# An attention and two-layer kernel: transposed tails moved behind the scores, reciprocal broadcasts re-ordered, a rounding moved from ScalarE to GpSimd, copies put ahead of exponentials

## What is computed

```python
# attention: 4 batches x 8 heads, 576 positions, head size 64
scores = q @ k.T / sqrt(64)
scores = where(scores >= max(scores) - tau, scores, -1e9)
attn = exp(scores - max(scores)); attn = attn / (sum(attn) + 1e-9)
x = attn @ v                      # heads side by side: 2304 tokens x 512
# two layers, each 512 -> 2048 -> 512
h = x @ w_in;  g = h * tanh(softplus(h));      x = g @ w_out
h = x @ w_in2; g = h * clip(h + 3, 0, 6) / 6;  out = g @ w_out2
```

## Time and profile before

| | |
|---|---|
| median of 3 runs | 1034.86 us (1034.7 to 1036.05) |
| the profiled execution, its own device time | 1034.37 us |
| its span, first to last instruction | 1032.6 us |
| PE busy | 1007.6 us, 98% of the span |
| DVE busy | 863.6 us, 84% |
| ACT busy | 638.3 us, 62% |
| POOL busy | 478.7 us, 46% |
| DMA engines, mean busy in attention | about 0.9 |

### The profile page before, as it was taken

How to read it: one execution, slowest core, us unless ns; L and a number is a source line. 1 busy time by engine, 2 the same in 40 slices (tenths; PEclk the granted TensorE clock), 3 DMA queues, 4 the chain that set the end, 5 groups by cost and what they waited for, 6 DMA issues and landing times.

```text
span 1032.6 us, 20134 instructions
## 1 busy us (share of the span) xinstructions
PE 1007.6 (98%) x6984; PEld 934.9 (91%) x6984; DVE 863.6 (84%) x1694; ACT 638.3 (62%) x1170; POOL 478.7 (46%) x515
## 2 busy tenths in 40 slices
PE   5999999999999999999999999999999999999998
PEld 4777777777778999999999999999999999999998
DVE  6888888888884899888997899877996779957884
ACT  5777777777874666555665566555564556555543
POOL 6865655757825740278005840178004850078200
PEclk9999999999999999999999999999999999999999
DMA  5699898889853899589894999553795357753664
GB/s 181 169 243 245 243 252 255 231 233 273 212 162 143 275 305 363 197 275 320 288 391 150 289 311 354 198 166 127 245 325 171 136 175 280 255 174 108 227 244 162
DMA packets 146083, 241.44 MB, mean 234 GB/s; under 512 B 11072, under 2 KB 79168, under 8 KB 145984
## 3 DMA queue, kind: packets, MB, share of 16 engines
q1 hardware_dynamic: 145984, 240.17, 72.7%
HBM read 164.76 MB, written 50.59 MB: 209 GB/s over the span
## 4 chain that ended last, share of the span: by engine, by line
PE 59%; DVE 7%; ACT 5%; issue 3%; DMA 1%; DVEq 0%; ACTq 0%
PE banks L803 7%; PE banks L805 7%; PE banks L804 7%; PE banks L840 6%; PE banks L839 6%; PE banks L838 6%; PE banks L846 5%; PE banks L848 5%; PE banks L847 5%; ACT relu L1034 3%; PE banks L726 1%; DMA ring<-w_out_mix 1%; DVE first_kept L1240 1%; ACT ring L999 1%; PE banks L672 1%
## 5 line engine op out<-in xcount | busy, mean ns | idle before, releaser
L1525 POOL TENSOR_TENSOR ring<-raw,ring 128x256 fp32r<-128x256 f32 x336 | 282.6, 877 | 386.6 <-ACT ring L999 386.6
L803 PE MATMUL banks<-x_high,ring 128*128 128x384 f32 x672 | 226.5, 337 | 1.3 <-issue 0.7
L805 PE MATMUL banks<-x_high,ring 128*128 128x384 f32 x672 | 224.8, 335 | 0.0
L804 PE MATMUL banks<-x_low,ring 128*128 128x384 f32 x672 | 224.7, 334 | 0.0
L839 PE MATMUL banks<-ring,g_high 128*128 128x256 f32 x504 | 142.6, 283 | 0.0
L840 PE MATMUL banks<-ring,g_low 128*128 128x256 f32 x504 | 142.6, 283 | 0.0
L838 PE MATMUL banks<-ring,g_high 128*128 128x256 f32 x504 | 142.6, 283 | 0.0
L932 ACT ACTIVATE exps<-banks,neg_max 128x576 f32<-128x576 f32 x144 | 107.2, 745 | 43.7 <-DVE neg_max L1187 42.5
L1161 DVE SCALAR_TENSOR_TENSOR probs<-banks,thresh,exps 128x576 f32<-128x576 f32 x144 | 117.2, 814 | 20.2 <-ACT exps L932 16.0
L803 PEld LDWEIGHTS banks<-x_high,ring 128*128 128x128 f32 x672 | 126.1, 188 | 6.6 <-issue 4.7
L804 PEld LDWEIGHTS banks<-x_low,ring 128*128 128x128 f32 x672 | 126.2, 188 | 0.0
(11 more groups left out here) (112 smaller groups left out, 2118.8 us busy)
## 6 DMA issues: line engine op xcount, KB each, us to landing
ring<-w_out_mix SPq DMA_DIRECT2D x168, 512.0 KB, 5.2
raw<-w_in_mix SPq DMA_DIRECT2D x48, 896.0 KB, 5.7
w_in_mix<-prep_in SPq DMA_DIRECT2D x18, 896.0 KB, 6.5
w_out_mix<-prep_high SPq DMA_DIRECT2D x16, 896.0 KB, 4.6
w_out_mix<-prep_low SPq DMA_DIRECT2D x16, 896.0 KB, 7.0
prep_in<-w_in SPq DMA_DIRECT2D x64, 128.0 KB, 3.4
prep_out<-w_out SPq DMA_DIRECT2D x64, 128.0 KB, 2.8
k_high<-k_two_high SPq DMA_DIRECT2D x56, 144.0 KB, 3.0
```

Of the source, the lines that this page charges most:

```text
L803: nc.tensor.matmul(dst, w[:, 0, cols], high, start=(t == 0 and m < 4), stop=False, skip_group_check=True)
L804: nc.tensor.matmul(dst, w[:, 0, cols], low, start=False, stop=False, skip_group_check=True)
L805: mm = nc.tensor.matmul(dst, w[:, 1, cols], high, start=False, stop=(t == KH - 1), skip_group_check=True)
L1525: nc.gpsimd.tensor_tensor(ring_slot(slot)[:, 1, :], raw[q % 2][:, m, :], f32(ring_slot(slot)[:, 0, :]), ALU.subtract).then_inc(w_low_ready, 1)
```

## The change

1. PE: the tail of tile t-2 is turned directly behind the second half of tile t's scores (`turn_tail`). In odd tiles that is ahead of the next tile's first half, in even tiles ahead of `mix`. The main blocks stay where they were.
2. PE: `spread_sums` makes the 64 columns of the shared tile first and signals them apart. ACT copies them ahead of tile 2's exponentials.
3. POOL now rounds the mixed weights in one instruction, and takes their rest in one instead of three; ACT's three roundings go.
4. ACT: in odd tiles the main blocks of tile t-2 are copied ahead of tile t's exponentials.
5. The first nine tiles get an order of their own, tile by tile: no look-ahead on PE, exponentials ahead of copies on ACT, and on DVE each tile's `weigh` behind the next tile's maximum.

```diff
@@ PE, attention_step
+                if t < PAIR_TILES:
+                    score_half(it, s, 0)
+                    score_half(it, s, 1)
+                    if t >= 2:
+                        turn_tail(t - 2, s - 2)
+                        turn(t - 2, s - 2)
+                    return
                 if even(i):
                     if i == 0:
                         score_half(it, s, 0)
                     score_half(it, s, 1)
+                    turn_tail(t - 2, (s - 2) % TILES_IT)
                     if i == SPREAD_AT and pair >= 0:
                         spread_sums(pair, b, t)
@@
                 else:
                     score_half(it, s, 0)
                     score_half(it, s, 1)
+                    turn_tail(t - 2, (s - 2) % TILES_IT)
 
                     score_half(it, s + 1, 0)
-                if t >= 2:
-                    turn(t - 2, (s - 2) % TILES_IT)
+                turn(t - 2, (s - 2) % TILES_IT)
@@ ACT, attention_step
-                if even(i):
-                    take_exp(t, s)
+                if even(i) and t >= PAIR_TILES:
                     if i == SPREAD_AT and pair >= 0:
                         keep_spread_tail(pair)
+                    take_exp(t, s)
@@
-                    take_exp(t, s)
-                    if t >= 2:
+                    if t >= PAIR_TILES:
                         keep_main(t - 2, (s - 2) % TILES_IT, pair2)
+                        take_exp(t, s)
+                    else:
+                        take_exp(t, s)
+                        if t >= 2:
+                            keep_main(t - 2, (s - 2) % TILES_IT, pair2)
@@ ACT, the loop over tiles
-                    if s >= 16 and it < ITS - 1:
-                        round_prep(0, it, s - 16)
-                    if s == 0 and it > 0:
-                        round_prep(0, it - 1, 2)
@@ DVE, attention_step
+                early = t < PAIR_TILES
+                if early and t > 0 or t == PAIR_TILES or even(i) and i > 0:
+                    weigh(t - 1, s - 1)
                 if i == 0 and pair >= 0:
                     take_recips(pair, b)
-                elif even(i) and i > 0:
-                    weigh(t - 1, s - 1)
@@
-                if even(i):
+                if even(i) and not early:
                     weigh(t, s)
@@ POOL
+            def round_prep(u):
+                pool.wait_ge(prep_out_mixed, 4 * u + 4)
+                after(pool, prep_out_stored, 32 * u)
+                words = prep_out[:, :, :].rearrange("p m n -> p (m n)")
+                nc.gpsimd.tensor_tensor(prep_high[:, :, :].rearrange("p m n -> p (m n)"), words,
+                                        one[:, :].to_broadcast([P, MIXES * WORDS]), ALU.mult).then_inc(prep_out_rounded, 1)
@@
                 if it + 1 < ITS:
                     split_two(it + 1, 0)
+                round_prep(it - 1)
                 rest_prep(it - 1)
```

More of the change, by code:

```diff
@@ L270, in attention_and_layers @@
         recips_ready = sem("recips_ready")
+        spread_tail_ready = sem("spread_tail_ready")
         spread_ready = sem("spread_ready")
@@ L381, in late_part @@
             return divmod(GROUPS * r + q, 3) if r < SPANS else (LATE_UNITS, q)
-        PREP_PARTS = (slice(0, 2), slice(2, 5), slice(5, MIXES))
+        PREP_PARTS = (slice(0, MIXES),)
         LATE_PARTS = (slice(0, 4), slice(4, MIXES))
@@ L675, in score_half, with turn_tail, turn @@
                     mm.then_inc(scores_ready, 1)
-            def turn(t, s):
-                pe.wait_ge(probs_ready, t + 1)
+            def turn_tail(t, s):
                 i, own = t % PAIR_TILES, probs_of(t)
                 if tail_first(i):
+                    pe.wait_ge(probs_ready, t + 1)
                     tail = own[:, 0:P] if i == PAIR_TILES - 1 else probs[:, i // 2 % 2, SEQ - TAIL:SEQ + TAIL]
                     nc.tensor.transpose(turned_tail[s % 3], tail, ident[:, :]).then_inc(tail_turned, 1)
+            def turn(t, s):
+                i, own = t % PAIR_TILES, probs_of(t)
+                pe.wait_ge(probs_ready, t + 1)
                 after(pe, main_kept, t)
@@ L696, in spread_sums @@
                 after(pe, x_ready, 2 * pair)
[L697 to L701, removed]
                 pe.wait_ge(probs_ready, t - 1)
@@ L706, in spread_sums @@
                                           ident[:, TAIL * a:TAIL * a + TAIL], start=True, stop=True)
+                mm.then_inc(spread_tail_ready, 1)
+                for i in range(MAIN):
+                    for a in range(2):
+                        col = a * (MAIN + 1) + i
+                        mm = nc.tensor.matmul(spread_main[DH * a:DH * a + DH, P * i:P * i + P], recips[:, b, col:col + 1].to_broadcast([P, DH]),
+                                              ident[:, :], start=True, stop=True)
                 mm.then_inc(spread_ready, 1)
@@ L859, in _ @@
             mix(ITS, last - 1, 1 - b, 1, MIX1_AT[0])
+            turn_tail(end - 2, TILES_IT - 2)
             turn(end - 2, TILES_IT - 2)
@@ L863, in _ @@
             up(0, 0, S3_T3)
+            turn_tail(end - 1, TILES_IT - 1)
             turn(end - 1, TILES_IT - 1)
@@ L919, in keep_spread_tail @@
             def keep_spread_tail(pair):
-                act.wait_ge(spread_ready, pair + 1)
+                act.wait_ge(spread_tail_ready, pair + 1)
                 nc.scalar.copy(spread[:, MAIN * P:SEQ], spread_tail(pair)).then_inc(spread_kept, 1)
             def keep_spread_main(pair):
+                act.wait_ge(spread_ready, pair + 1)
                 nc.scalar.copy(spread[:, 0:MAIN * P], spread_main).then_inc(spread_kept, 1)
@@ L1492, in mix_prep_out @@
                     nc.gpsimd.tensor_tensor(prep_out[:, to, :], prep_out[:, a, :], prep_out[:, b, :], op).then_inc(prep_out_mixed, 1)
+            def round_prep(u):
[4 more added lines that the diff above has]
+                                        one[:, :].to_broadcast([P, MIXES * WORDS]), ALU.mult).then_inc(prep_out_rounded, 1)
             def rest_prep(u):
[L1496 to L1499, removed]
+                pool.wait_ge(prep_out_rounded, u + 1)
+                nc.gpsimd.tensor_tensor(prep_low[:, :, :], prep_out[:, :, :], f32(prep_high[:, :, :]),
+                                        ALU.subtract).then_inc(prep_out_split, 1)
             def mix_x(n):
```

## The result

| | before | changed |
|---|---|---|
| median of all runs, 20 of each | 1037.7 us (1034.7 to 1041.02) | 1035.1 us (1030.59 to 1037.19) |
| ratio to before, 95% interval | | 0.9970 (0.9959 to 0.9982) |
| profiled execution, its span | 1034.37, 1032.6 us | 1033.87, 1032.0 us |

The changed kernel is faster by 0.30%, 3.1 us, with an interval from 1.9 to 4.2. The prediction started from three runs with the median 1034.86; the 17 further runs of the kernel before lie between 1035.26 and 1041.02, so its plain median is higher. Applied to 1034.86, the ratio gives 1031.8; the prediction said 1031.5. The two profiled executions lie only 0.5 us apart. So the traces are read for what happens in attention, and the ratios for the time.

A forecast was written before the change was run, and what follows sets the result against it. PE was taken to bound attention, with SP's DMA chain limiting what is kept: 2.8 (rounding at s = 6) + 0.1 (odd tiles) + 0.5 (first weights) = 3.4 us, so 1031.0, median 1031.5 us; range 1028.6 to 1035.

The forecast's parts named there:

- a PE that gains far more than is kept: Attention: PE alone would gain 10.8 us, but SP's DMA deliveries at their old times let only 3.4 be kept.
- 2.8 us at ACT's rounding at s = 6: Last iteration: ACT's rounding comes at most 2.8 us earlier, since it also waits for placed keys landing at 282.87.
- +0.08 for each odd tile: PE, odd tiles: the added step from transposes to scores costs 0.08 of the 0.10 us saved; 0.1 us a pair net.
- Copies ahead of the exponentials: ACT, odd tiles: exponentials start later and DVE's weigh waits 0.2 us, but PE has cover; taken at nothing.
- (b): Thin cover: exponentials exceed it by 0.05 to 0.12 us per odd tile; 1032.5 to 1033.9 us; chance 0.22.
- (c): Slower: odd tiles' exponentials later than worked out; at 0.25 us beyond the cover, 1039 us; chance 0.13.
- POOL: Rounding on POOL takes 3.6 us, bounded by 0 and 4.3; SP is not delayed, 0 at either bound.
- The first nine tiles: Start of attention: DVE and ACT take 1.7 us a tile instead of 1.9, about 2.4 us by tile 11.
- Within 1 us of the old ones: SP's issue times up to 300 us stay within 1 us of those in the kernel before.
- The hold at the values: PE's mix at tile 4 of pairs 4, 6, 8, 10 and 12 waits for values; at most 0.3 us ahead at pair 9's.
- ACT's waits for POOL go: Rounding on POOL removes ACT's three roundings and its waits for POOL; no size was given.
- Rival (d): The clock: a longer PE wait for a transfer brings back slow product spacing; one such stretch gives 1033.5 us; chance 0.05.

The follow-up runs named there:

- pe_tail: The kernel before with PE's tails alone moved directly behind the scores: 1035.63 us, ratio 0.9991.
- pool_round: The kernel before with the rounding of mixed weights alone moved to POOL, without ACT's three roundings: 1034.45 us, ratio 0.9973.
- after_values: The changed kernel with odd pairs' values loaded ahead of the next queries and keys and the store of mixed weights: 1024.86 us, ratio 0.9887.
- act_copy: The kernel before with only ACT's main-block copies put ahead of the odd tiles' exponentials, from tile 9 on: 1036.39 us, ratio 0.9997.
- after_no_pool: The changed kernel with ACT rounding the mixed weights again in three pieces and POOL's rest in three: 1035.93 us, ratio 0.9998.
- before_values: The kernel before with odd pairs' values loaded ahead of the next load of queries and keys: 1034.45 us, ratio 0.9980.
- fewrows pair: The kernel before and the changed kernel, each with placing DMAs cut to 16 of 128 rows: 1034.4 and 1021.23 us, ratios 0.9983 and 0.9857.

## Why the prediction was right

The time, the sign and the size were right, and the picture of a PE that gains far more than is kept. The sum behind the size was not: its largest term, 2.8 us at ACT's rounding at s = 6, didn't happen, and the gain came from a step that it left without a price. That 3.4 us stood there and 3.1 were measured is luck. Point by point:

**The tail.** The step "+0.08 for each odd tile" was wrong. The rows of PE in tile 5 of the changed kernel's period 7:

```profile
147.95 0.28 PE L673 MATMUL banks<-k_low,q_stack 128*128 128x256 f32 x1
148.07 0.27 PE L684 MATMUL banks<-ident,probs 128*128 128x128 f32 x1
148.10 0.36 PE L673 MATMUL banks<-k_high,q_stack 128*128 128x256 f32 x1
148.30 0.28 PE L673 MATMUL banks<-k_low,q_stack 128*128 128x256 f32 x1
148.47 0.63 PE L694 MATMUL banks<-ident,probs 128*128 128x128 f32 x4
```

The next product starts 0.03 us behind the tail, and the one after it 0.20 later: 0.23 together, as much as a tail (0.11) and a product (0.12) took before. I had charged the slow step behind a transpose and not taken off the transpose's own shorter spacing. So the whole 0.10 goes in four tiles, and the floor fell by 0.56 instead of 0.1 us a pair. pe_tail alone shows 0.39 of it and pool_round 0.07; what the other 0.10 is made of no run takes apart.

**Copies ahead of the exponentials.** Right. ACT's exponentials of tile 5 now start 0.58 us behind the maximum's end at 149.03, and DVE's `weigh` waits 0.21 us for them; PE doesn't wait.

```profile
149.61 0.75 ACT L950 ACTIVATE exps<-banks,neg_max 128x576 f32<-128x576 f32 x1
...
150.40 0.82 DVE L1179 SCALAR_TENSOR_TENSOR probs<-banks,thresh,exps 128x576 f32<-128x576 f32 x1 [0.21 <-ACT exps L950]
```

With that the rivals (b) and (c) fall.

**POOL.** 3.17 us for the rounding, where 3.6 was taken, and 4.02 for the rest in one instruction where three took 4.30. SP wasn't delayed by it: its last load of queries starts at 249.34 in the changed kernel and 250.01 in pool_round, and at 249.98 to 250.68 in pe_tail, act_copy and after_no_pool, where POOL does not round (247.18 in the kernel before). What was not priced is the lock: one 4 us instruction instead of three of up to 1.8 can hold DVE's small operation longer, 1.32 us at 61.49 in the changed kernel and 2.37 in after_values; the three hold it at most 1.09 us in the kernel before and 1.69 in before_values.

**The first nine tiles.** 2.4 us forecast, 1.76 in the two profiled executions, 2.4 in the fewrows pair. No run has this part alone; the first `spread_sums` starts at 29.60 to 30.76 in the seven traces with the old order and at 26.93 to 28.36 in the seven with the new one.

**SP's times.** "Within 1 us of the old ones" failed: SP issues the fifth iteration's load of queries at 195.94 against 193.19. That the change moved it isn't needed to explain this: with POOL as before, pe_tail has it at 194.66, act_copy at 195.62 and after_no_pool at 195.68; pool_round has it at 197.47. The profiled execution of the kernel before had the earliest chain of all with this order on SP and whole placing DMAs. The prediction took one execution's landings as fixed; with the same code on SP and POOL they lie up to 2.5 us apart here. How much of that is chance, no second trace of the same kernel shows.

**What is kept.** The hold at the values was foreseen for periods 4, 6, 8, 10 and 12; it came in 4, 8 and 12, and in 6 and 10 only the weight loads waited, 0.2 and 0.4 us. The hold at ACT's rounding at s = 6 never came: it stands directly behind the copy,

```profile
284.65 0.59 ACT L925 COPY probsT<-banks 128x512 f32<-128x512 f32 x1
285.13 0.84 ACT L1008 CAST x_high<-x 128x768 fp32r<-128x768 f32 x1
```

0.54 us ahead of its old time and not 2.8. In the profiled execution the wait for values until 241.06 had put PE behind its old place (240.66), and the first `up` came 0.88 us earlier instead of 3.4. So the sum of 3.4 was the right size for another reason than the one it gives. It set the change against an execution in which ACT hardly waited for POOL (2.3 us), while its relatives with that code show 2.4 to 12.4 us. The reading that fits all runs is that this hold was replaced by the one at the values, which binds a few microseconds later; it is argued, since the kernel before has one trace. The step itself, that ACT's waits for POOL go, stands in the prediction without a price; by pool_round and after_no_pool it is, within the intervals, the whole measured gain.

**Rival (d).** Chance 0.05, and it happened, twice in the profiled execution, for 1.67 and 1.38 us. The waits were longer than forecast; PE was faster than forecast and the chain later. The Trainium skill (TensorE: Matmul & The Clock Gate, Part 1) has the engine fall to half its clock by idling; the windows above show exactly that, and here also in the granted clock.

## What to carry to other kernels

Where an engine works beside a chain of DMAs of nearly its own length (35.5 against 37.4 us an iteration here), a faster engine keeps only the lead of the chain; look for the chain's idle gaps and put into them what the engine will next wait for. One move in SP's order, worth 2 us to the kernel before, turned a gain of 3 us into one of nearly 12. And take the slack of a delivery from several traces: the one execution shown can be the one in which the hold is absent.

## What the runs showed of the hardware

- A DVE operation on 128x9 that takes 0.16 us alone took up to 2.37 us and ended within 0.03 us of the end of a 4.02 us POOL instruction. Divided into pieces of at most 1.8 us, the same work held it 1.57 us at most. A DVE operation on 128x1 beside the same POOL instructions took its usual 0.21 us.
- Waits of PE of 4.08 and 3.18 us (values) were followed by some 3.4 and 2.7 us of work at a granted clock of 0.50, and cost 1.67 and 1.38 us beyond themselves; one of 1.85 us was not.
- One 128x128 transpose between products costs nothing beyond its 0.11 us: the slow start of the product behind it (0.20) is made up by the short step ahead of it (0.03).
- In four kernels with the same code on SP and POOL, but not on PE and ACT, one execution each, the same DMA of SP's chain was issued at 193.19, 194.66, 195.62 and 195.68 us.
